# Second batch of a fused attention and mixture-of-experts kernel: w2 by seven products of quarters, splits of w1 and gated weights through DRAM

## The reference, cut to what matters

```
a = attention(q, k, v)             # 2 batches, 768 tokens each, 512 channels
p = domain_probs / (sum + 1e-9)    # 4 gates for each token
for e in range(4):                 # w1: 512x1024, w2: 1024x512, f32
    h = maximum(x @ w1[e], 0)
    out += p[:, e:e+1] * (h @ w2[e])
h = (out @ w1g) * (out @ w2g) @ w3 # gated stage, 512x1024 twice, 1024x1024
y = h @ w_out                      # 1024x512 (w3 @ w_out is folded beforehand)
```

## Time and profile before

| | us |
|---|---|
| median of 3 runs | 826.4 |
| lowest run | 824.42 |
| highest run | 995.0 |
| profiled execution, its own time | 825.13 |
| its span, first to last instruction | 822.9 |

### The profile page before, as it was taken

One profiled execution on the slowest core, in us unless ns is written; L12 is line 12 of the kernel. 1 busy time (PEld: TensorE's weight loads), 2 busy tenths in 40 slices (PEclk: granted clock), 3 DMA queues, 4 the chain that ended last, 5 costly groups with the idle time before them and its releaser, 6 DMA issues.

```text
span 822.9 us, 12913 instructions
## 1 busy us (share of the span) xinstructions
PE 807.1 (98%) x4798; PEld 762.4 (93%) x4798; DVE 409.3 (50%) x907; ACT 328.1 (40%) x627; POOL 546.8 (66%) x464
## 2 busy tenths in 40 slices
PE   9999988999999999999999999999999999999998
PEld 7667767999999999999899899999999999999987
DVE  6875676513534533635666364154354345366620
ACT  4477783532431431533343354143144134234411
POOL 3488996693783783775795797845835835939820
PEclk9999999999999999999999999999999999999999
DMA  8933462232312312310233233222222222202202
GB/s 300 364 108 127 182 222 78 80 100 71 103 52 71 103 52 70 104 52 25 68 120 101 97 109 116 77 76 81 69 71 78 77 71 78 67 12 77 78 2 78
DMA packets 25363, 79.59 MB, mean 97 GB/s; under 512 B 3264, under 2 KB 4560, under 8 KB 25296
## 3 DMA queue, kind: packets, MB, share of 16 engines
q1 hardware_dynamic: 20912, 70.16, 25.1%
q10 hardware_dynamic: 4320, 8.52, 3.0%
q0 software_dynamic: 64, 0.03, 0.2%
HBM read 71.85 MB, written 6.84 MB: 96 GB/s over the span
## 4 chain that ended last, share of the span: by engine, by line
PE 88%; POOL 5%; DVE 4%; ACT 1%; DMA 1%; issue 1%; DVEq 0%; SPq 0%; ACTq 0%
PE bank L50 28%; PE bank L52 28%; PE bank L51 28%; POOL pr L490 2%; PE bank L602 1%; PE bank L619 1%; PE bank L592 1%; POOL bl L1094 1%; DMA fold_mt_raw<-m3t 1%; DVE fold_wo_l L204 0%; ACT pr L497 0%; DVE bias_tmp L419 0%; DVE bias_w L396 0%; DVE bias_tmp L382 0%; DVE bias_tmp L411 0%
## 5 line engine op out<-in xcount | busy, mean ns | idle before, releaser
L50 PE MATMUL bank<-bh,ah 128*128 128x384 f32 x672 | 225.3, 335 | 2.5 <-DVE parts L1533 1.3
L52 PE MATMUL bank<-bh,al 128*128 128x384 f32 x672 | 224.5, 334 | 0.0
L51 PE MATMUL bank<-bl,ah 128*128 128x384 f32 x672 | 224.5, 334 | 0.0
L50 PE MATMUL bank<-hh,w2h 128*128 128x384 f32 x512 | 171.0, 334 | 0.0
L51 PE MATMUL bank<-hl,w2h 128*128 128x384 f32 x512 | 171.0, 334 | 0.0
L52 PE MATMUL bank<-hh,w2l 128*128 128x384 f32 x512 | 171.0, 334 | 0.0
L1035 POOL TENSOR_TENSOR al<-raw,ah 128x512 fp32r<-128x512 f32 x96 | 122.0, 1291 | 70.4 <-ACT ah L1015 69.6
L1048 POOL TENSOR_TENSOR w2l<-raw,w2h 128x1024 fp32r<-128x1024 f32 x40 | 96.2, 2411 | 104.9 <-ACT w2h L1043 104.2
L50 PEld LDWEIGHTS bank<-bh,ah 128*128 128x128 f32 x672 | 126.1, 188 | 4.7 <-DVE parts L1533 1.9
L51 PEld LDWEIGHTS bank<-bl,ah 128*128 128x128 f32 x672 | 126.2, 188 | 0.1
L52 PEld LDWEIGHTS bank<-bh,al 128*128 128x128 f32 x672 | 126.1, 188 | 0.0
(11 more groups left out here) (118 smaller groups left out, 1166.2 us busy)
## 6 DMA issues: line engine op xcount, KB each, us to landing
raw<-weights SPq DMA_DIRECT2D x80, 512.0 KB, 3.5
k<-k SPq DMA_DIRECT2D x8, 704.0 KB, 6.8
v<-v SPq DMA_DIRECT2D x8, 704.0 KB, 4.4
raw<-folded SPq DMA_DIRECT2D x8, 512.0 KB, 3.8
fold_mt_raw<-m3t SPq DMA_DIRECT2D x7, 512.0 KB, 8.4
q<-q SPq DMA_DIRECT2D x8, 384.0 KB, 4.7
out<-rows ACTq DMA_DIRECT2D x11, 256.0 KB, 2.1
gate<-gates ACTq DMA_DIRECT2D x7, 384.0 KB, 3.8
```

The source lines that it names most:

```text
L50: nc.tensor.matmul(out, wh, xh, start=start, stop=False, skip_group_check=adds_on)
L51: nc.tensor.matmul(out, wh, xl, start=False, stop=False, skip_group_check=adds_on)
L52: return nc.tensor.matmul(out, wl, xh, start=False, stop=stop, skip_group_check=adds_on)
```

## The change

In batch 1 (`t == 1`) the w2 products go by seven products of quarters too. An expert's w2 is now four *down pieces* n0 to n0 + 3, each with the four quarters and three sums of a pair of 128-row blocks; two output groups j = 2e (pieces n0, n0 + 1) and j + 1 (pieces n0 + 2, n0 + 3) do seven products D1 to D7 of 4 x 3 matmuls (`down_group`), in the order D1, D6, D2, D7, D5, D4, D3. `second_expert` starts j's products while the last up group ends. The hidden activations' four sums T1 to T4 are made for each up group by DVE (`rectified_sum`, from PSUM), rounded by ACT (`sum_high`) and split by POOL (`sum_low`, 384 columns each); T1 and T2 lie in `b_sum`, T3 and T4 in `raw[2]`. Down pieces take turns with the up groups in the same three slots, and go through `down_sums` (POOL, four of 256 columns), `down_high` (ACT) and `down_low` (POOL) in four parts: A11 with A12, S1 with S2, A22 with S3 (512 columns each), S4 (256). `kept_high` and `kept_low` split the three quarters that are kept, `add_x` takes the place of `drain` (two DVE operations a block, one for the first expert), `down_snap` copies D1's bank.

In batch 0, SP stores the split weights of each of the 24 up groups to DRAM (`store_split`, two transfers, 1.84 MB a group). In batch 1, `load_splits` brings them back (1.84 MB a group, six transfers) in place of the raw weights; `up_sums`, `up_high` and `up_low` are gone there. The sums of the tokens for the last gated stage are made in portions of 384 columns, and the first products of that stage go in another order (P1, half of P5 and of P6, P2, P1 and P2 of the next group, then the other halves). The diff, cut:

```diff
+PARTS = ((A11, A12), (S1, S2), (A22, S3), (S4,))
+LOADS = (A11, A12), (A22, S3), (S1, S2, S4)
+DOWN_ORDER = (1, 6, 2, 7, 5, 4, 3)
+DOWN_SUMS = ("u2", "u3", "c22", "c21", "c12")
...
+    def store_split(self, sp, g):
+        s, rows = self.slot(g), slice(g * P, (g + 1) * P)
+        sp.wait_ge(self.a_raw_low, g + 1)
+        sp.wait_ge(self.a_sum_low, g + 1)
+        for part, t in enumerate((self.ah[s], self.al[s])):
+            sp.dma_start(self.splits[rows, part * OPS * QUART:(part + 1) * OPS * QUART],
+                         t[:, :].bitcast(F32)).then_inc(self.split_stored[s], 16)
+    def load_split(self, sp, i, p):
+        s, g, r = self.slot(i), i - UPS, self.ring(i) - 3
+        if r < UPS:
+            sp.wait_ge(self.p3, r + 1)
+            sp.wait_ge(self.split_stored[s], 32 * (UPS // 3))
+        elif r < UPS + E * PER_EXPERT and (r - UPS) % PER_EXPERT >= KH:
+            e, n = divmod(r - UPS, PER_EXPERT)
+            sp.wait_ge(self.dn_product, self.dn_count(DOWNS * e + (n - KH) // 2, (2, 4, 3)[p]))
+        else:
+            e, n = divmod(r - UPS, PER_EXPERT)
+            sp.wait_ge(self.p3, UPS + (KH * e + n if e < E else r - UPS - KH * E) + 1)
...
+    def load_splits(self, sp, *groups):
+        for p in range(len(LOADS)):
+            for i in groups:
+                self.load_split(sp, i, p)
...
+        down = self.at("down", 0)
+        self.load_splits(sp, UPS)
+        self.load_splits(sp, UPS + 1)
+        self.load_splits(sp, UPS + 2)
+        self.load_piece(sp, down)
+        self.load_piece(sp, down + 1)
+        for e in range(E):
+            i0, m = UPS + KH * e, down + 4 * e
+            self.load_splits(sp, i0 + 3)
+            self.load_piece(sp, m + 2)
+            self.load_piece(sp, m + 3)
+            self.load_splits(sp, i0 + 4)
+            self.load_piece(sp, m + 4)
+            self.load_piece(sp, m + 5)
+            self.load_splits(sp, i0 + 5, i0 + 6)
...
+            act.wait_ge(self.split_stored[self.slot(g)], 32 * (g // 3))
...
+    def down_sums(self, pool, n):
...
+        self.wait_raw(pool, "down", n)
+        if n:
+            pool.wait_ge(self.dn_low, len(PARTS) * n)
+        else:
+            pool.wait_ge(self.a_sum_low, UPS)
+        nc.gpsimd.tensor_tensor(s1, a21, a22, ALU.add).then_inc(self.dn_step, 1)
+        pool.wait_ge(self.dn_step, c + 1)
+        nc.gpsimd.tensor_tensor(a21, a21, a11, ALU.subtract).then_inc(self.dn_step, 1)
+        nc.gpsimd.tensor_tensor(s2, s1, a11, ALU.subtract).then_inc(self.dn_step, 1)
+        pool.wait_ge(self.dn_step, c + 3)
+        nc.gpsimd.tensor_tensor(s4, a12, s2, ALU.subtract).then_inc(self.dn_step, 1)
...
+    def down_high(self, act, n, p):
+        src, to = self.down_part(n, p)
+        e, j = divmod(n, 2 * DOWNS)
+        if j < 2 * DOWNS - 1:
+            act.wait_ge(self.p3, UPS + KH * e + j + 2)
+        else:
+            act.wait_ge(self.dn_product, self.dn_count(DOWNS * e, (2, 5, 4, 3)[p]))
+        self.wait_raw(act, "down", n)
+        if p:
+            act.wait_ge(self.dn_step, 4 * n + 4)
+        self.nc.scalar.activation(self.ah[self.slot_down(n)][:, to], src, ACT.Copy).then_inc(self.dn_high, 1)
+    def down_low(self, pool, n, p):
+        src, to = self.down_part(n, p)
+        s = self.slot_down(n)
+        pool.wait_ge(self.dn_high, len(PARTS) * n + p + 1)
+        self.nc.gpsimd.tensor_tensor(self.al[s][:, to], src, self.ah[s][:, to].bitcast(F32),
+                                     ALU.subtract).then_inc(self.dn_low, 1)
...
+    def down_group(self, pe, j, p, ks=range(KH)):
+        nc, (e, d) = self.nc, divmod(j, DOWNS)
+        a, b, c, start = {1: (A11, B11, 11, True), 6: (S2, T2, 21, True), 5: (S1, T1, 12, True), 2: (A12, B21, 11, False),
+                          7: (S3, T3, 21, False), 4: (A22, T4, 21, False), 3: (S4, B22, 12, False)}[p]
+        if 0 in ks:
+            if start:
+                self.bank_free(pe, UPS + KH * e + 2 + d, c)
+            elif p == 2:
+                pe.wait_ge(self.dn_snapped, j + 1)
+            else:
+                pe.wait_ge(self.dn_sum, self.sum_count(j, {7: "u2", 4: "u3", 3: "c22"}[p]))
+        out = self.bank[3 * d + (11, 21, 12).index(c)][:, 0:TT]
+        for k in ks:
+            i, n = UPS + KH * e + k, 2 * j + k // 2
+            s = self.slot_down(n)
+            pe.wait_ge(self.dn_low, len(PARTS) * n + [a in part for part in PARTS].index(True) + 1)
+            if b >= T1:
+                pe.wait_ge(self.t_low, self.t_count(i, b))
+            else:
+                pe.wait_ge(self.h_low[{B11: 11, B21: 21, B22: 22}[b]], self.h_count(i) + 1)
...
+            if k == KH - 1:
+                last.then_inc(self.dn_product, 1)
+    def second_expert(self, pe, e):
+        i0 = UPS + KH * e
+        for i in range(i0, i0 + KH):
+            if i > i0:
+                self.product4(pe, i - 1)
+                self.product3(pe, i - 1)
+            else:
+                self.product1(pe, i)
+            self.product6(pe, i)
+            self.product5(pe, i)
+            self.product2(pe, i)
+            self.product7(pe, i)
+            if i < i0 + KH - 1:
+                self.product1(pe, i + 1)
+        j = DOWNS * e
+        self.down_group(pe, j, 1, (0, 1))
+        self.product4(pe, i0 + 3)
+        self.product3(pe, i0 + 3)
+        self.down_group(pe, j, 1, (2, 3))
+        self.down_group(pe, j, 6, (0, 1, 2))
+        self.down_group(pe, j, 5, (0, 1))
+        self.down_group(pe, j, 2, (0, 1))
+        self.down_group(pe, j, 6, (3,))
+        self.down_group(pe, j, 2, (2, 3))
+        self.down_group(pe, j, 7)
+        self.down_group(pe, j, 5, (2, 3))
+        self.down_group(pe, j, 4)
+        self.down_group(pe, j, 3)
+        for p in DOWN_ORDER:
+            self.down_group(pe, j + 1, p)
...
+    def sum_high(self, act, i, b):
+        act.wait_ge(self.t_made, self.t_count(i, b))
+        self.nc.scalar.activation(self.sh[b][i % KH][:, :], self.t_raw(b), ACT.Copy).then_inc(self.t_high, 1)
...
+    def second_expert_scalar(self, act, e):
+        i0, n0 = UPS + KH * e, 4 * e
+        for g in range(KH):
+            i = i0 + g
+            if g or e:
+                self.snap(act, i)
+            if g:
+                self.kept_high(act, i - 1, 22)
+                self.kept_high(act, i - 1, 21)
+                self.keep_h11(act, i - 1)
+                if g >= 2:
+                    self.down_high(act, n0 + g - 2, 0)
+                self.sum_high(act, i - 1, T1)
+                self.sum_high(act, i - 1, T2)
+            if g == 0:
+                self.gate_load(act, E + e)
+            self.kept_high(act, i, 11)
+            if g:
+                self.sum_high(act, i - 1, T3)
+                self.sum_high(act, i - 1, T4)
+            if g >= 2:
+                for p in range(1, len(PARTS)):
+                    self.down_high(act, n0 + g - 2, p)
+        self.kept_high(act, i, 22)
+        self.kept_high(act, i, 21)
+        self.keep_h11(act, i)
+        self.down_snap(act, DOWNS * e)
+        for b in (T1, T2, T3, T4):
+            self.sum_high(act, i, b)
+        for n in (n0 + 2, n0 + 3):
+            for p in range(len(PARTS)):
+                self.down_high(act, n, p)
+        self.down_snap(act, DOWNS * e + 1)
...
+    def sum_low(self, pool, i, b):
+        k = i % KH
+        pool.wait_ge(self.t_high, self.t_count(i, b))
+        if b == T4 and k:
+            for s in range(2):
+                pool.wait_ge(self.y_stored[s], 16 * (ROWS_OUT // 2))
+        self.nc.gpsimd.tensor_tensor(self.sl[b][k][:, :], self.t_raw(b), self.sh[b][k][:, :].bitcast(F32),
+                                     ALU.subtract).then_inc(self.t_low, 1)
+    def sums_low(self, pool, i):
+        for b in (T1, T2, T3, T4):
+            self.sum_low(pool, i, b)
+    def second_expert_gpsimd(self, pool, e):
+        i0, n0 = UPS + KH * e, 4 * e
+        self.sums_low(pool, i0)
+        self.down_low(pool, n0, 0)
+        self.sums_low(pool, i0 + 1)
+        for p in range(1, len(PARTS)):
+            self.down_low(pool, n0, p)
+        self.down_low(pool, n0 + 1, 0)
+        self.down_sums(pool, n0 + 1)
+        self.sums_low(pool, i0 + 2)
+        for p in range(1, len(PARTS)):
+            self.down_low(pool, n0 + 1, p)
+        self.sums_low(pool, i0 + 3)
+        for n in (n0 + 2, n0 + 3):
+            self.down_sums(pool, n)
+            for p in range(len(PARTS)):
+                self.down_low(pool, n, p)
+        if e < E - 1:
+            self.down_sums(pool, n0 + 4)
...
+    def rectified_sum(self, dve, i, b):
+        c = {T1: 12, T2: 22, T3: 11, T4: 21}[b]
+        less = {T1: self.s1[i % 2][:, :], T2: self.t_raw(T1), T3: self.t_raw(T2), T4: self.t_raw(T2)}[b]
+        q = self.t_count(i, b)
+        if b == T1:
+            dve.wait_ge(self.kept, self.h_count(i) - KH * E + 1)
+            dve.wait_ge(self.c12_made, i + 1)
+        else:
+            dve.wait_ge(self.t_made, self.t_count(i, min(b - 1, T2)))
+        if q > 4:
```

(46 more changed lines are left out.)

480 lines of the change are left out of this document (369 added, 111 removed).

## The result

The changed kernel takes 850.0 us (median of four runs) beside 825.9 us: a ratio of 1.031, 95% interval 1.027 to 1.035. One of the four executions of before took 995.0 us, far above the other three, and is not in the ratio. The profiled execution of after took 854.38 us with a span of 852.8; its mean granted clock was 0.981, where the other four had 0.988 or 0.989 and 849.3 to 850.8 us.

What follows compares the result with a forecast made beforehand. PE's work was taken as the bound, with POOL's list adding waits: 825.1 - 16.6 (removed matmuls) + 4 x 8.1 (experts) + 1 (stores) + 0.8 (gated stage start) = 842.7, so 843 us; range 826 to 855.

Steps and rivals of the forecast that it cites:

- The gain of 16.6 us: Batch 1's experts: 96 fewer w2 matmuls on PE at 0.1728 us each, 2.0% of 825.1 us.
- The path through POOL: Each expert: POOL's 35.9 us list, begun at 16.8 us from a freed slot, makes PE wait; expert 66.2 us.
- 2.7, 1.4 and 4.0: PE's waits in us per expert: D6's third block, D6's last block (T2), third block of D1 in j + 1.
- Rivals 1 and 2: Experts: POOL's work hidden, 810 us, chance 0.10; or POOL faster and partly hidden, 826 to 836 us, chance 0.15.
- Rival 3: Up groups: DVE's loop exceeds 7.26 us or ACT's block reaches it, 3 us an expert, 855 us; chance 0.07.
- Rival 4: Batch 0: stores delay raw pieces by more than POOL's idle time, 16 us, 858 us; chance 0.05.
- the 1 us that I took for them: Batch 0's stores in SP's queue between loads: cost taken as 1 us, bounds 0 and 4 us.
- Rival 5: Experts: PE's clock falls in the new gaps, 2 us lost after each expert's gap, 8 us, 851 us; chance 0.06.
- the 842 us from which I called it slower: Whole kernel: above 842 us counts as slower by over 2%; chance of that 0.51.
- The loads "at 0": Batch 1's loads of split weights land before they are needed, cost 0; gated stage at 324 GB/s, under 406.
- 4 x 8.1 - 16.6: Four experts: each 8.1 us over its new ideal of 58.1 us, less the 16.6 us of removed matmuls.
- The start of the last gated stage: Next group's snap on ACT at about 4.8 us, P2 due at 4.1 us; cost taken as 0.8 us.

Runs made afterwards that it cites:

- e10: Changed kernel with POOL's work partly moved to DVE in order of need, plus ACT's copy of D1's bank two operations earlier: 820.22 us, 0.9941 of before.
- e2: Changed kernel with POOL's low part of T4 done twice, four more operations in each expert: 866.37 us, 1.0501 of before.
- e5: Changed kernel with T1 to T4's low parts of each expert's last up group moved from POOL to DVE: 834.22 us, 1.0107 of before.
- e7: Changed kernel with POOL's second part of n0 + 1 earlier and PE taking D2's third block before D6's: 855.06 us, 1.0364 of before.
- e6: Changed kernel with 20 useless matmuls put into PE's wait ahead of D1's third block of j + 1: 844.62 us, 1.0238 of before.
- e4: Changed kernel with SP issuing loads ahead of the raw pieces in the last gated stage: 848.3 us, 1.0281 of before.
- e1: Kernel before with only batch 0's stores of split weights added, nobody reading them: 824.67 us beside 824.89, 0.9997.
- e9: Changed kernel with POOL work moved to DVE, PE, ACT and DVE in order of need, SP's loads ahead of raw pieces: 822.39 us, 0.9973 of before.
- e3: Changed kernel with POOL's low parts of T1 to T4 cut to 64 of 384 columns: 826.02 us, 1.0026 of before.
- e8: Changed kernel with SP's loads first, T parts on DVE, D6's waits merged, half of the last two w2 pieces' low parts on DVE: 841.17 us, 1.0188 of before.

## Why the prediction was right, and what it missed

**The gain of 16.6 us is there as less work for PE**, whose pace stayed 0.173 us a matmul. No run has shown it whole: the best, e10, has its experts 7.8 us under before, at 60.1 us where one without any wait would take 58.1.

**The path through POOL was right, step by step.** First part at 16.85 (forecast 16.8), `sum_low` 1.011 us (taken 1.0 between 0.75 and 1.255), the list's end at 52.3 (52.7). The gaps in the second expert's starts, less a matmul each, are 2.4, 1.25 and 3.7 us, 7.4 in all, against 2.7, 1.4 and 4.0, 8.1. That these waits come from the length of the list is shown by lengthening it (e2: its end 3.2 us later for three operations more, PE's expert 3.35 us longer) and shortening it (e5: its end 2.65 us earlier, PE's expert 4.7 us shorter, of which 2 us are the clock's). That it is one budget and not three faults is shown by e7.

**Rivals 1 and 2 (POOL hidden, or fast) are out** by the waits. **Rival 3 (DVE's loop) is out**: PE waits for DVE in no expert of after. **Rival 4** is out by the stores alone; the 1 us that I took for them is 0.

**Rival 5 was no rival but a term that was missing.** A wait of PE in this kernel has a second price, matmuls at half clock behind it. I gave it a chance of 0.06 as an alternative, though its condition, a gap of some 4 us, was part of my own forecast. It was to be added: 8 us was my price, and e6 measures 7.7 us in the experts of the profiles and at most 5.4 in the medians. The 851 us of that rival are also nearer to the measured 850.0 than the 843 are. Without the clock the kernel would have been at the edge of the 842 us from which I called it slower, so that it is clearly slower is owed to the term that I had left out.

**The loads "at 0" were mis-sized by SP's order.** In the experts it holds. In the last gated stage I checked bytes and slots, but not that a load stands behind a raw piece which itself waits for POOL. In the profiles that is 3.6 us (e4), in the medians 1.7.

**What is left is the forecast.** By stages, from the profiles, against before: experts 264.3 - 249.6 = 14.7 us (e6, forecast 4 x 8.1 - 16.6 = 15.8), last gated stage 60.8 - 59.7 = 1.1 (e4, forecast 0.8), the stores 0 (e1, forecast 1), the end 1.7 (forecast 0). That is 17.5 us against 17.6, and so close only by luck: the end, which the forecast didn't have, makes up for the stores and for what the experts came out cheaper. No run has e4's and e6's edits alone together, and since e6's gated stage is shorter too, their medians can't simply be added.

**The start of the last gated stage** has waits of 0.71 (ACT's snap, taken at 0.8) and 1.39 for a low part on DVE (`hl`), which I hadn't seen as late. e9 still has the latter, with 1.4 as its longest.

**Open:** the 1.7 us behind the last output row. From the last output row's copy on ACT to the end of the span before takes 822.9 - 819.0 = 3.9 us, after 852.8 - 847.2 = 5.6. The other kernels with the changed second batch have it too, the stores alone don't; no run tells which of its parts does it. Open too is most of why the profiled execution of after had a lower clock than the four others and took 4 us more. One fall of it, in the attention, is seen above and goes with the 1.0 us by which batch 1 starts later; that how many matmuls are slow behind one and the same wait varies is seen in e3.

## What to carry to other kernels

When the bound engine gets less work, take a helper engine's list in order from the event that lets it begin (here a freed slot) to each operand that the bound engine needs; its average busy share tells nothing, and one more microsecond in such a list costs a whole one. Add the clock's price behind the last wait of such a list instead of keeping it as another scenario; ahead of a further wait it is hidden. Expect work that is moved to DVE to slow POOL while it runs, if both its operands are in SBUF. If the list is too long, move work by order of need and look at each queue on the way (SP's as well), since a helper with idle time but a wrong order only hands the wait on: e8 and e9 move the same work, 841.2 and 822.4 us.

## What the runs showed of the hardware that I had not expected

- After most gaps of 2.2 to 4.8 us between PE's starts, up to 17 matmuls run 0.32 to 0.33 us apart instead of 0.173, some from the first one behind the gap on, some only from the third to the ninth. A gap of the same length (2.45 us, e3) had 11 and 10 such matmuls behind it in two experts and none in two; of after's four gaps of 2.6 us at D6, only the first expert's had any. Whether a gap costs is therefore not a matter of its length alone here. Filling it with 20 useless matmuls took the fall away (e6).
- DVE's subtraction of two SBUF operands and POOL's work can slow each other: DVE, 384 columns, 1.03 us against the 0.54 to 0.56 of operations with an operand in PSUM; POOL, 256 columns, 1.04 against 0.73. In e9 the same DVE operation of 512 columns took 0.68 us in the four cases where POOL stood idle and 1.11 to 1.34 in nine beside POOL. In three more it took 0.68 beside POOL, and POOL's low part of 256 columns took 1.27 instead of 0.73. Two of the sixteen:

```profile
516.19 0.68 DVE L1208 TENSOR_TENSOR al<-raw,ah 128x512 fp32r<-128x512 f32 x1
518.35 1.23 DVE L1208 TENSOR_TENSOR al<-raw,ah 128x512 fp32r<-128x512 f32 x1 [1.01 <-ACT ah L1201]
```

  The Trainium skill, SBUF — State Buffer, section "Who interferes with whom", says that a DVE instruction with two SBUF inputs contends with a GpSimd instruction that reads SBUF, and that one with at most one such input doesn't, outside the modes in which DVE uses two ports. The rows above agree with the first half. For the second, DVE's sums with an operand in PSUM kept to 0.54 to 0.57 us in e9, with POOL busy beside them or not. The earlier trace rows had shown POOL's side of it before the prediction.
- The stores of batch 0 to DRAM, beside loads, cost nothing that can be measured (e1: 0.9997, 0.9988 to 1.0006).
